# Squares of the third and fourth batch added by GpSimd's DMA queue, and the last batch's weight loads issued at other places of ScalarE's queue

## What is computed

```
mag = np.sqrt(a_re * a_re + a_im * a_im)
scale = np.minimum(mag, 0.999) / (mag + 1e-06)
a_re_n, a_im_n = (a_re * scale, a_im * scale)
...
new_re = ar * S_re - ai * S_im
new_im = ar * S_im + ai * S_re
S_re, S_im = (new_re + kv, new_im)
y[:, :, t] = np.einsum('bhd,bhde->bhe', q[:, :, t], S_re)
```

## Time and profile before

| what | us |
| --- | --- |
| median of 3 runs | 611.38 |
| the 3 runs | 609.99, 611.38, 617.66 |
| the profiled execution, its own time | 613.04 |
| its span in the profile | 611.3 |
| mean granted TensorE clock of it | 0.941 of full |

### The profile page before, as it was taken

The page is one execution under the profiler, slowest core; times in us unless marked ns, Lnnn a source line. Parts: engine busy times, 40 slices in busy tenths (PEclk is TensorE's granted clock), DMA queues, the critical chain, the costliest instruction groups (busy, mean ns, idle before and its releaser), DMA issues.

```text
span 611.3 us, 11739 instructions
## 1 busy us (share of the span) xinstructions
PE 525.0 (86%) x4572; PEld 394.0 (64%) x4572; DVE 393.0 (64%) x651; ACT 336.0 (55%) x590; POOL 138.6 (23%) x118
## 2 busy tenths in 40 slices
PE   1430569997989798999899998999999999999997
PEld 1210247765667466766787644588888888888886
DVE  5899999999988999796542440599433233233322
ACT  6864624895548942275334312776556555555653
POOL 7000000000000000000000000266655555555553
PEclk9685679996989989999999998999999999999999
DMA  7400656558956488776679999200101001010101
GB/s 274 154 1 0 157 170 144 129 102 217 197 128 156 94 190 272 182 196 130 174 201 259 420 424 423 95 0 2 53 1 53 0 1 51 2 53 1 53 1 51
DMA packets 41607, 79.59 MB, mean 130 GB/s; under 512 B 7376, under 2 KB 29008, under 8 KB 40400
## 3 DMA queue, kind: packets, MB, share of 16 engines
q1 hardware_dynamic: 36944, 65.86, 37.6%
q10 hardware_dynamic: 4608, 12.99, 6.6%
HBM read 55.12 MB, written 4.72 MB: 98 GB/s over the span
## 4 chain that ended last, share of the span: by engine, by line
PE 59%; DVE 20%; ACT 7%; DMA 6%; issue 4%; SPq 2%; ACTq 1%; DVEq 0%
PE ps L1498 10%; PE ps L1494 10%; PE ps L1495 10%; PE ps L1201 8%; DMA stk<-xout 5%; PE ps L1187 3%; PE ps L1468 3%; DVE tt L858 3%; DVE big L864 3%; DVE tt L860 3%; SPq L277 2%; DVE big L832 2%; PE ps L1388 2%; PE ps L1410 2%; DVE xout L954 2%
## 5 line engine op out<-in xcount | busy, mean ns | idle before, releaser
L1166 DVE TENSOR_TENSOR qs<-rs 128x512 f32<-128x512 f32 x96 | 82.6, 860 | 118.9 <-ACT rs L727 118.9
L788 POOL TENSOR_TENSOR hlo<-qs,hhi 128x512 fp32r<-128x512 f32 x96 | 126.3, 1316 | 128.8 <-DVE qs L1166 124.8
L1494 PE MATMUL ps<-hhi,who 128*128 128x512 f32 x285 | 111.0, 389 | 0.0
L1495 PE MATMUL ps<-hhi,wlo 128*128 128x512 f32 x285 | 110.9, 389 | 0.0
L727 ACT ACTIVATE rs<-ps 128x512 f32<-128x512 f32 x96 | 57.4, 597 | 82.3 <-PE ps L1468 82.1
L1187 PE MATMUL ps<-ident 128*32 128x512 bf16 x256 | 74.0, 405 | 31.3 <-DVE xout L954 31.3
L1201 PE MATMUL ps<-stk 112*128 112x224 f32 (+1 forms) x384 | 81.8, 371 | 15.2 <-DMA stk<-xout 15.1
L1201 PEld LDWEIGHTS ps<-stk 112*128 112x128 f32 x384 | 72.6, 206 | 27.2 <-DMA stk<-xout 20.7
L1498 PE MATMUL ps<-hlo,who 128*128 128x512 f32 x285 | 80.5, 390 | 0.1
L780 POOL MEMSET sinz<- 128x768 f32 x1 | 0.7, 738 | 328.1 <-PE ps L1244 328.1
L731 ACT ACTIVATE hhi<-rs 128x512 fp32r<-128x512 f32 x96 | 60.8, 633 | 3.1
(11 more groups left out here) (161 smaller groups left out, 813.8 us busy)
## 6 DMA issues: line engine op xcount, KB each, us to landing
stk<-xout SPq DMA_DIRECT2D x132, 128.0 KB, 3.7
wt<-in_w SPq DMA_DIRECT2D x8, 1536.0 KB, 19.0
big<-in_a_all SPq DMA_DIRECT2D x12, 768.0 KB, 5.3
xq<-in_xq SPq DMA_DIRECT2D x24, 384.0 KB, 4.8
wt<-in_w ACTq DMA_DIRECT2D x12, 768.0 KB, 7.3
vr<-in_v_all SPq DMA_DIRECT2D x24, 192.0 KB, 4.6
out<-ost SPq DMA_DIRECT2D x5, 768.0 KB, 3.5
wins<-in_w_in SPq DMA_DIRECT2D x1, 3072.0 KB, 25.0
```

Source lines behind the costliest of these rows:

```text
L788: pool.tensor_tensor(hlo[:, i % NHS, :], qs[:, i % NQS, :], hhi[:, i % NHS, :].bitcast(F32), ALU.subtract).then_inc(lo_ready, 1)
L1166: dve.tensor_tensor(qs[:, i % NQS, :], rs[:, i % NQS, :], rs[:, i % NQS, :], ALU.mult).then_inc(sq_ready, 1)
L1494: nc.tensor.matmul(accs[k], wh[k], hi, start=(f == 0), stop=False)
L1495: nc.tensor.matmul(accs[k], wl[k], hi, start=False, stop=False)
```

## The change

The sums U_ + V_ of batches 2 and 3 are made by six DMAs of GpSimd's queue whose write adds to the destination (accum_op). Each waits for the two squares of its part, and each part has a semaphore of its own; `log_m2` waits for it. VectorE's `norm2` stays for batch 0 alone, and the six calls for the later batches go, with the `fill` ahead of four of them. In pass 4 the weight loads of ScalarE's queue move from behind the restack of turn n + 1 to the start of the turn c, ahead of the exponentials and of `copy_kt`; halves 9, 10 and 11 move a turn further ahead as well (from c = 3, 4, 5 to c = 2, 3, 4), and nothing is loaded at c = 5.

```diff
@@ log_m2 (ScalarE)
-                    act.wait_ge(m2_ready, DT * (b - (b > 1)) + t + 1)
+                    if b:
+                        act.wait_ge(m2_added[t], 16 * (b - 1))
+                    else:
+                        act.wait_ge(m2_ready, t + 1)
                     x = u = grid(U_ + t * PT, [1, PT])
@@ ScalarE's passes, ahead of take_squares, exponentials and copy_kt
+                    if p == B and c == 1:
+                        act.wait_ge(chain, C_ALL * B)
+                        act.wait_ge(kq_ready, 2 * NC * (B - 1))
+                        load_part(6, 3, 4)
+                        load_part(10, 0, 2)
+                    elif p == B and c == 2:
+                        load_half(8)
+                        load_half(9)
+                    elif p == B and c == 3:
+                        load_half(10)
+                        load_part(5, 0, 2)
+                    elif p == B and c == 4:
+                        load_half(11)
+                        load_part(5, 2, 3)
@@ ScalarE's passes, behind stack(n + 1)
-                    if p == B and c == 1:
-                        act.wait_ge(chain, C_ALL * B)
-                        act.wait_ge(kq_ready, 2 * NC * (B - 1))
-                        load_part(6, 3, 4)
-                    if p == B and 2 <= c < NC:
-                        load_half(NC + c)
-
-                    if p == B and c == 1:
-                        load_part(10, 0, 2)
-                    if p == B and c == 3:
-                        load_part(5, 0, 2)
-                    if p == B and c == 4:
-                        load_part(5, 2, 3)
@@ GpSimd, behind the constants
+            for b in range(2, B):
+                for t in range(DT):
+                    pool.wait_ge(squares, DT - 1 + 2 * (DT * (b - 1) + t + 1))
+                    pool.dma_start(grid(U_ + t * PT, [1, PT]), grid(V_ + t * PT, [1, PT]), accum_op=ALU.add).then_inc(m2_added[t], 16)
@@ VectorE: norm2
-            def norm2(b, t):
-                if b == 0:
-                    dve.wait_ge(squares, min(t + 1, DT - 1))
-                    dve.wait_ge(own_squares, t + 1 + (t == DT - 1))
-                else:
-                    dve.wait_ge(squares, DT - 1 + 2 * (DT * (b - 1) + t + 1))
+            def norm2(t):
+                dve.wait_ge(squares, min(t + 1, DT - 1))
+                dve.wait_ge(own_squares, t + 1 + (t == DT - 1))
@@ VectorE's passes
-                    if 0 < p < B - 1 and 1 <= c < 3:
-                        fill(p)
-                        norm2(p + 1, c - 1)
...
-                    if 0 < p < B - 1 and c == 2:
-                        norm2(p + 1, 2)
```

More of the change, by code:

```diff
@@ L199, in program @@
         kv_done, s_copied, y_done = sem("kv_done"), sem("s_copied"), sem("y_done")
-        m2_summed = sem("m2_summed")
+        m2_summed, m2_added = sem("m2_summed"), [sem(f"m2_added{t}") for t in range(DT)]
         y_copied, x_done, x_copied = sem("y_copied"), sem("x_done"), sem("x_copied")
@@ L1020, in _ @@
                 first_squares(t)
-                norm2(0, t)
+                norm2(t)
             for t in range(DT):
```

## The result

| | median us | runs | ratio to before |
| --- | --- | --- | --- |
| before | 611.08 | 6 (609.33 to 617.66) | |
| changed | 618.60 | 6 (615.03 to 623.22) | 1.0134, 95% interval 1.0101 to 1.0168 |
| changed, once more (after_again) | 621.59 | 6 (616.57 to 626.58) | 1.0147 (1.0092 to 1.0201) |

What follows compares the result with a forecast made beforehand. No engine was taken to bound throughout: VectorE early in passes 1 and 2, then restacks and TensorE, with ScalarE's queue in pass 4. Terms +3.1 - 2.4 - 3.9 = -3.2 took 611.38 to 608.2 us, range 602.8 to 614.0.

Steps and rivals of the forecast that it cites:

- VectorE's additions: Passes 1 and 2: 5.2 us of VectorE work go, only one of six additions on the path, so -0.9 us.
- rival 3: Added DMAs find gaps; without the slow clock at the 170.0 stop 1.5 more goes: 602.7 to 604.2 us; chance 0.15.
- The adding DMAs: Passes 1 and 2: three transfers delay restacks on the path, 1.2 us each: +1.2, +2.4, and +0.4 for low clock.
- The loads ahead: Pass 4: loads at turn start mostly done before ScalarE's restack DMAs, last restack 8.56 to about 5 us: -2.4 at turn 23.
- Rival 2: Pass 4: loads ahead in ScalarE's queue hold back the restack, turns 20 to 22 about 1 us later each: 612; chance 0.2.
- Rival 1: Passes 1 and 2: an adding transfer costs 5.2 us of engine time, delaying restacks 4 and 6.5 us: 615.2; chance 0.17.
- The issues ahead of copy_y: Pass 4: load issues at c = 1, 2, 3 (1.1, 0.6, 1.1 us) delay copy_y, which TensorE awaits; moving them removes this.
- The experts' part: wt[14] lands about 5.5 us earlier; the 2.43 us stop ahead of hidden(3) goes and its product takes 2.78: -3.9 us.
- The sum: Whole kernel: +3.1 (passes 1 and 2) - 2.4 (pass 4) - 3.9 (experts' part) = -3.2 us.

Runs made afterwards that it cites:

- no_add: Kernel before with the six additions of V_ to U_ for batches 2 and 3 left out, no DMA in their place, loads as before: ratio 0.9960.
- accum_late: As accum_only, but each adding DMA also waits until the restack it met before has landed: ratio 0.9999 to the kernel before.
- amount_only: Kernel before with the halves of pass 4's weight loads moved a turn ahead, all loads still behind ScalarE's restack DMAs: ratio 0.9952.
- plain_copy: As accum_only, but GpSimd's six DMAs copy V_ over U_ instead of adding: ratio 0.9985 to the kernel before.
- accum_only: Kernel before with GpSimd's six adding DMAs in place of VectorE's additions, weight loads where they were: ratio 1.0116.
- accum_again: accum_only run once more, unchanged, on one chip with the whole change and its other half: 616.54 us, ratio 1.0071 to the kernel before.
- loads_on_pool: Kernel before with the changed kernel's pass 4 loads issued by GpSimd instead of ScalarE; VectorE adds as before: ratio 1.0120.
- loads_only: Kernel before with pass 4's weight loads moved as in the changed kernel, VectorE's additions as before: ratio 1.0139.
- amount_spread: As amount_only, with ScalarE's loads of pass 3 one half per turn: 607.81 us, ratio 0.9947 to the kernel before.
- loads_again: loads_only run once more, unchanged: 616.24 us, ratio 1.0079 to the kernel before.

## Why the prediction was wrong, step by step

- *VectorE's additions, -0.9.* Right in kind: not all of the 5.2 us of work lies on the path. no_add measured -2.4, interval -4.7 to -0.2, which holds -0.9 as it holds the clock that I had put into rival 3. A mask does wait longer: the second one of turn 1, reached at 94.2 us in no_add, accum_late and amount_only alike, waits 1.50 and 1.56 us in the first two and not at all in amount_only, where VectorE still adds.
- *The adding DMAs, 1.2 us each.* The place was right for turn 1: its restack is held up by the transfer that I named, while the latency is hidden (no logarithm waits for it). The size failed. From the two nearest rows, 1.0 and 2.6, I took a value near the first because the tile's rows are as long as a load's. That is the price of a copy (1.1, plain_copy); an adding transfer takes 2.2. On turn 1 the traces give the price directly, +2.0 to +2.5, against +1.1 with copies. With a price of 2 x 1.0 us the sum of both passes had been +5.5, and accum_only costs 7.1 us in one group (1.16%) and 4.3 as accum_again (0.71%). The Trainium skill ("Collectives: The Full Stack", The bandwidth ceiling) says that an adding DMA needs two source reads and ran at half the speed of a copy; the traces agree with the factor of two, and show no reads. For turn 8, which was to take two of the three transfers, nothing is shown: against turn 7 it is later by 2.5 us in the changed trace and by 0.4 in accum_only, and earlier in the two repeated ones. So of the 4.3 to 7.1 us, the 2.0 to 2.5 of turn 1 are located, the rest isn't; and plain_copy, at the price that I had assumed, measured -0.9 where the sum says +3.1. The sum was wrong beyond its price.
- *The loads ahead, -2.4.* This is the step that gave the wrong sign. I wrote that the loads "are mostly done when ScalarE's three restack DMAs are issued", from the share of 0.21 at 318 to 320 us. That stretch lies ahead of turn 22. Ahead of turn 20 the kernel before had a share of 0.73 and 0.78 already, from the other three restack DMAs and the next inputs. The new place of the loads lies at about 296.8 us of this trace, and ScalarE's three restack DMAs of turn 20 go out at 300.29. In the 4 us from 296 to 300 about 1 us of all engines is free, by my estimate 0.4 MB at the 402 GB/s of the earlier trace rows; 1.2 MB more didn't fit. The gap of 0.21 comes behind. Turn 20 began 2 us late (2.1 to 4.2 in the six traces with loads ahead); then the low clock added 2.7 us to its products, and turns 22 and 23 stopped again. The sum from turn 18 to 23 is +4.6 to +8.8 in place of -2.4. Rival 2 named this mechanism, with a chance of 0.2, but priced it at 1 us per turn, without the clock, and gave the queue's order as the cause; loads_on_pool shows that another queue doesn't help. Rival 1 came nearest in time (615.2) by a wrong price: it wanted 5.2 us per adding transfer.
- *The issues ahead of copy_y, 1.1 us on three turns.* They went, and it didn't matter, since the restack became the later one. amount_only keeps them and is faster.
- *The experts' part, -3.9.* Right in every row: no stop, 2.78 us for the product, wt[14] in time, and 3.9 us measured from turn 23 to the end in loads_only. That it was the bytes alone isn't shown by this number, since TensorE comes 15.2 us late there. amount_only and amount_spread show it better: at turn 23 they are 1.7 and 0.5 us late, and the stop is 0.57 us and none. How much of the 3.9 in the late traces is due to the bytes stays open.
- *The sum.* +3.1 - 2.4 - 3.9, with its first two terms put right, is about +5.5 + 6 - 3.9 = +7.6, and 7.5 was measured. That agreement is luck: part by part it fails. The loads' share would be +6 - 3.9 = +2.1, and loads_only costs 8.5, loads_again 4.8. In the trace of loads_again 2.8 of the 3.4 us are there at turn 18 already, ahead of everything that this part changes.

What stays open is where the rest of each part's cost lies, and why turn 14 waits 1.96 us for its restack in one trace and 11.13 in another, with the same loads in pass 3. It may be behind much of the spread between executions. The one kernel that changed these loads, amount_spread, had the shortest wait (1.26 us) in its one trace, but no measurable gain over amount_only.

## What to carry to other kernels

Before a transfer is moved ahead "into a gap", look at the DMA share from its new issue until the next urgent transfer lands, not at the emptiest stretch nearby; what is under way at that moment delays the urgent one, whichever queue it came from, so bulk loads belong behind it, not ahead of it. That is no full protection: amount_spread, with its loads behind, still stopped for 1.50 and 2.02 us at turns 22 and 23. An addition that is handed to a DMA cost twice the engine time of a copy here (2.2 against 1.1 us for 0.39 MB), and none of these kernels shows it paying: beside restacks on the path it lost, away from them (accum_late) it changed nothing. And a stop of TensorE has to be priced with the low clock that can follow it, which at turn 20 cost nearly as much as the stop.

## What the runs showed that I had not expected

Taking the loads out of the urgent DMAs' queue gave these no protection: with the loads on GpSimd's queue the restack of turn 20 landed 8.54 us after its last issue (one trace), with them ahead in ScalarE's own 5.96 to 7.27 (five traces). A stop of 3.02 us on turn 20 was followed by 2.7 us of loss at the low clock, nearly doubling it; behind the stop of 1.12 us on turn 22 the products took 3.29 us, as without a stop. And two executions of one kernel differ by 6 us at turn 11 with no difference in their program: a single trace sizes no effect of a few us, though it shows each one's place.
